# Attention in groups of 64 tokens, two tokens to a row, in units of two batches and half the heads

## The reference

```python
# r, k, v: (4 batches, 8 heads, 768 tokens, 48), w, u: (8, 48)
for t in range(S):                                   # linear attention with a decaying state
    kt, vt, rt = (k[:, :, t], v[:, :, t], r[:, :, t])
    cur = np.einsum('bhd,bhe->bhde', u[None] * kt, vt)
    y[:, :, t] = np.einsum('bhd,bhde->bhe', rt, state + cur)
    state = w[None, :, :, None] * state + np.einsum('bhd,bhe->bhde', kt, vt)
x = y.transpose(0, 2, 1, 3).reshape(B * S, H * D)    # 3072 x 384
# soft mixture of experts: 8 experts, 4 slots each
logits = x @ phi                                     # 3072 x 32
d = softmax over the tokens; slot_input = d.T @ x    # 32 x 384
slot_out[e] = np.maximum(slot_input[e] @ w1[e], 0.0) @ w2[e]
x = softmax over the slots of logits @ slot_out
# feed-forward: elu between two matrices
h = x @ w_in                                         # 3072 x 2048
g = np.where(h > 0.0, h, np.exp(np.minimum(h, 0.0)) - 1.0)
out = g @ w_out                                      # 3072 x 384
```

## Time and profile before

| | |
|---|---|
| median of 3 runs | 399.86 us (398.61 to 400.44) |
| profiled execution | 397.44 us, its span 395.7 us |
| PE busy | 377.8 us, 95% of the span |
| DVE, ACT, POOL busy | 267.8, 220.0, 105.1 us |
| DMA | 87,280 packets, 51.80 MB; 77,776 packets under 512 bytes |
| chain that ended last | PE 77%, SP's queue 12%, DMA 3%, issue 3% |

### The profile page before, as it was taken

One profiled execution on the slowest core, in us unless ns is written; L12 is line 12 of the kernel. 1 busy time (PEld: TensorE's weight loads), 2 busy tenths in 40 slices (PEclk: granted clock), 3 DMA queues, 4 the chain that ended last, 5 costly groups with the idle time before them and its releaser, 6 DMA issues.

```text
span 395.7 us, 11454 instructions
## 1 busy us (share of the span) xinstructions
PE 377.8 (95%) x4379; PEld 335.1 (85%) x4379; DVE 267.8 (68%) x514; ACT 220.0 (56%) x499; POOL 105.1 (27%) x136
## 2 busy tenths in 40 slices
PE   6898999999969999999999999999999999999997
PEld 3787898988855453489999999999999999999996
DVE  3787788777756820499966776677767776677671
ACT  2796778777763140468664446444654465455541
POOL 5897877777640000146400000000000000000000
PEclk9999999999999999999999999999999999999999
DMA  9998899999999999830011002000200020002002
GB/s 173 226 170 187 179 224 230 236 258 253 257 328 432 396 385 404 328 80 2 0 36 47 2 0 80 0 0 0 80 0 0 0 80 0 0 0 81 1 2 80
DMA packets 87280, 51.80 MB, mean 131 GB/s; under 512 B 77776, under 2 KB 83024, under 8 KB 85200
## 3 DMA queue, kind: packets, MB, share of 16 engines
q1 hardware_dynamic: 82912, 50.40, 42.9%
q10 hardware_dynamic: 4336, 0.98, 1.3%
HBM read 45.86 MB, written 4.72 MB: 128 GB/s over the span
## 4 chain that ended last, share of the span: by engine, by line
PE 77%; SPq 12%; DMA 3%; issue 3%; DVE 2%; POOL 2%; ACT 0%; POOLq 0%; DVEq 0%
PE psum L969 17%; PE psum L971 17%; PE psum L970 16%; PE psum L905 6%; SPq L367 5%; SPq L369 3%; PE psum L836 3%; SPq L368 3%; PE psum L817 3%; DMA r_raw<-in_r_dram 3%; PE psum L594 2%; PE psum L634 2%; PE psum L677 2%; PE psum L687 1%; PE psum L658 1%
## 5 line engine op out<-in xcount | busy, mean ns | idle before, releaser
L971 PE MATMUL psum<-w_out_hi,elu_lo 128*128 128x384 f32 x372 | 125.8, 338 | 0.0
L969 PE MATMUL psum<-w_out_hi,elu_hi 128*128 128x384 f32 x372 | 125.7, 338 | 0.0
L970 PE MATMUL psum<-w_out_lo,elu_hi 128*128 128x384 f32 x372 | 125.3, 337 | 0.0
L1398 ACT ACTIVATE exp_h<-psum 128x512 f32<-128x512 f32 x96 | 57.7, 601 | 100.5 <-PE psum L905 100.4
L1245 DVE SCALAR_TENSOR_TENSOR elu<-psum,neg_part 128x512 f32<-128x512 f32 x96 | 66.2, 690 | 57.1 <-ACT neg_part L1385 57.1
L970 PEld LDWEIGHTS psum<-w_out_lo,elu_hi 128*128 128x128 f32 x372 | 69.8, 188 | 3.8
L969 PEld LDWEIGHTS psum<-w_out_hi,elu_hi 128*128 128x128 f32 x372 | 70.4, 189 | 0.0
L971 PEld LDWEIGHTS psum<-w_out_hi,elu_lo 128*128 128x128 f32 x372 | 69.9, 188 | 0.0
L1237 DVE TENSOR_TENSOR elu_lo<-elu,elu_hi 128x512 fp32r<-128x512 f32 x96 | 67.0, 698 | 0.6
L1279 ACT ACTIVATE scores<-ident_wide,bonus 128x128 f32<-128x128 f32 x192 | 58.8, 389 | 6.1 <-DVE bonus L1021 5.9
L1385 ACT ACTIVATE neg_part<-exp_h 128x512 f32<-128x512 f32 x96 | 59.9, 626 | 1.7 <-DVE elu L1245 1.3
(11 more groups left out here) (158 smaller groups left out, 410.7 us busy)
## 6 DMA issues: line engine op xcount, KB each, us to landing
w<-in_moe_w_dram SPq DMA_DIRECT2D x8, 1536.0 KB, 10.5
w_sb<-in_moe_w_dram SPq DMA_DIRECT2D x8, 1024.0 KB, 6.0
out_dram<-out_sb SPq DMA_DIRECT2D x24, 192.0 KB, 1.9
w_sb<-in_moe_w_dram SPq DMA_DIRECT2D x8, 512.0 KB, 6.4
w_out_raw<-in_moe_w_out_dram SPq DMA_DIRECT2D x4, 768.0 KB, 12.4
r_raw<-in_r_dram SPq DMA_DIRECT2D x12, 192.0 KB, 3.2
r_raw<-in_r_dram SPq DMA_DIRECT2D x24, 96.0 KB, 3.7
w_in_sb<-in_moe_w_in_dram SPq DMA_DIRECT2D x1, 2304.0 KB, 17.2
```

The source lines that it names most:

```text
L969: pe.matmul(acc, hi, w_out_hi[:, f, :], start=(f == 0), stop=False)
L970: pe.matmul(acc, hi, w_out_lo[:, f, :], start=False, stop=False)
L971: m = pe.matmul(acc, lo, w_out_hi[:, f, :], start=False, stop=(f == KF2 - 1))
L1398: act.activation(exp_h[:, f % 2, :], banks[4 + f % RING][:, :], ACT.Exp).then_inc(exp_done, 1)
```

## The change

Chunks stay at 128 tokens, units at 24. What a unit is changes: two batches of one chunk and four of the eight heads (`pr` is the pair of batches, `half` the half of the heads). A partition row holds two neighbouring tokens of one batch, 64 rows for each of the two batches, so a row of a transfer is 2 x 48 numbers, 384 bytes, and `load` issues two DMAs instead of three. Inside a chunk each batch is cut into two groups of 64 tokens, 32 rows each; with two batches there are four groups in a unit, one for each quarter of the partitions (`GROUPS`, `GROUP` = 32). Scores are 64 x 64 tokens per group and head, half as many elements as before. The second group of a batch must then see a state that has the first group in it: `state_mid`, made by DVE from the old state and the first group's key values (`state_middle`), and `state_sum` for the chunk's end (`state_end`).

Since tokens 2i and 2i+1 lie in one row, sums over tokens are two matmuls, one for each (`q`), and since a group has 32 rows its matmuls use tiles of 32 rows or 32 columns. `key_values`, `attend` and `values` are 32 matmuls a unit each, `state_in` comes in two parts of 8. r is turned by 16 matmuls with the identity on tiles of 64 rows (`turn_raw`) instead of 4 transposes, and waits for its part of PSUM; k is turned by 4 transposes as before. PSUM is laid out anew: banks 0 to 3 hold y and the key values, one bank for each group, 4 and 5 hold the turned r and the scores, 6 k, 7 x.

The diagonal moves from ACT to DVE (`diagonals`, one product of 512 columns), the copy of x from DVE to ACT, the decay from POOL to ACT (`decayed`). The copy of y on ACT is two instructions. The rows of the output lie two tokens apart, and each block of 128 is stored with two DMAs. The experts and the feed-forward stage have the same instructions on other banks.

```diff
+        GROUP = HP // 2
+        Q = 2
+        HALF_H = H // 2
...
-        v_sb = place("v_sb", [P, 2, B, H // 2, HP], F32)
-        scores = place("scores", [P, 2, H, P], F32)
+        v_sb = place("v_sb", [P, 2, H, Q * D], F32)
+        scores = place("scores", [P, 2, 2, 2, Q, HP], F32)
...
-        LOADED = 3 * 16
+        LOADED = 2 * 16
...
-        def load(eng, out, x, c, g, loaded):
-            bs, t0 = slice(2 * g, 2 * g + 2), c * P
-            even, odd = (x[rev, bs].rearrange("b t i d -> t b i d") for rev in range(2))
-            eng.dma_start(out[:, 0, bs, :, 0:D], even[t0:t0 + P]).then_inc(loaded[g], 16)
-            eng.dma_start(out[0:HP, 1, bs, :, 0:D], odd[t0 + HP:t0 + P]).then_inc(loaded[g], 16)
-            eng.dma_start(out[HP:P, 1, bs, :, 0:D], odd[t0:t0 + HP]).then_inc(loaded[g], 16)
+        def load(eng, out, x, c, pr, loaded):
+            for b in range(2):
+                eng.dma_start(out[b * HP:b * HP + HP, pr], x[2 * pr + b, c]).then_inc(loaded[pr], 16)
...
+            def turn_raw(out, raw, pr, half):
+                for a in range(2):
+                    for q in range(Q):
+                        for b in range(2):
+                            for two in range(2):
+                                rows = slice(b * HP, b * HP + HP)
+                                m = pe.matmul(out[rows_of(two), b, Q * a + q, :],
+                                              raw[rows, pr, head(half, two, a), q * D:(q + 1) * D],
+                                              ident[rows, rows], start=True, stop=True, skip_group_check=True)
+                return m
...
+                for a in range(2):
+                    for q in range(Q):
+                        for g in range(GROUPS):
+                            for two in range(2):
+                                rows, toks = rows_of(two), slice(g * GROUP, (g + 1) * GROUP)
+                                m = pe.matmul(ps_A[toks, two, a, q * HP:(q + 1) * HP], k_pair[rows, half, a, q, toks],
+                                              r_pair[rows, half, a, :, toks], start=True, stop=True,
+                                              skip_group_check=True)
+                m.then_inc(A_done, 1)
...
+            def key_values(un, pr, half, c, last):
...
+                pe.wait_ge(v_loaded[pr], LOADED * (c + 1))
+                wait_for(pe, yT_ready, un)
+                pe.nop(nofuse=True)
+                for a in range(2):
+                    for q in range(Q):
+                        for g in range(0, GROUPS, 2 if last else 1):
+                            for two in range(2):
...
+            def state_in(un, b, half, first, last, part):
+                if part == 0:
+                    pe.wait_ge(mid_ready, un + 1)
+                    if not first:
+                        pe.wait_ge(state_ready, un - B + 1)
+                    if not last:
+                        pe.wait_ge(state_summed, un + 1)
+                else:
+                    pe.wait_ge(inter_half_done, un + 1)
...
+            def values(un, pr, half, first):
+                pe.wait_ge(scores_ready, un + 1)
+                pe.wait_ge(inter_done, un + 1)
...
-                        key_values(un, b, i, c, 2 if first and b == 0 else un + 1)
-                    if not (first and b == 0) and not (last and b == B - 1):
-                        turn_k(un + 1, 1 - i, un + 2)
-                        turn_r(un + 1, (b + 1) % B, c + (b + 1) // B)
...
+                        turn_k(un + 1, 1 - half)
+                    key_values(un, pr, half, c, last)
...
+                        turn_r(un + 1, (b + 1) % B // 2, 1 - half, c + (b + 1) // B)
+                    state_in(un, b, half, first, last, 0)
+                    if not (first and b == 0):
+                        turn_x(un - 1, (b - 1) % B // 2, 1 - half)
...
+                    state_in(un, b, half, first, last, 1)
+                    values(un, pr, half, first)
+                    if not final:
+                        attend(un + 1, 1 - half)
...
+            def state_end(un):
+                dve.wait_ge(mid_ready, un + 1)
+                wait_for(dve, state_ready, un)
+                dve.tensor_tensor(state_sum[:, :, :, :].rearrange("p b a d -> p b (a d)"),
+                                  state_mid[:, un % 2].rearrange("p b a d -> p b (a d)"), ps_kv[:, 1], ALU.add
+                                  ).then_inc(state_summed, 1)
```

More of the change, by code:

```diff
@@ L498, in _ @@
[L498 to L502 removed]
+            pool.memset(phi_sb[:, :, :], 0.0).then_inc(cleared, 1)
+            pool.memset(k_nat[:, :, :, :, :, D:HP], 0.0).then_inc(pads_set, 1)
@@ L626, in attend @@
                 pe.nop(nofuse=True)
-                for cols, first in ((slice(0, P), 0), (slice(HP, P), 1)):
-                    for n in range(2):
-                        for two in range(2):
-                            for half, a in ((0, n + 2 * first), (1, n + 2 - 2 * first)):
-                                rows, e0 = slice(two * HP, two * HP + D), half * HP
-                                m = pe.matmul(ps_A[two][e0:e0 + HP, a, cols], k_pair[rows, i, a, e0:e0 + HP],
-                                              r_pair[rows, i, a, cols], start=True, stop=True, skip_group_check=True)
@@ new lines, in state_in @@
+            def state_in(un, b, half, first, last, part):
[5 more added lines that the diff above has]
+                        pe.wait_ge(state_summed, un + 1)
+                else:
+                    pe.wait_ge(inter_half_done, un + 1)
+                pe.nop(nofuse=True)
+                for s in ((1,) if first else (0, 1)):
+                    for a in range(2):
+                        for two in range(2):
+                            batch = two if part == 0 else 1 - two
+                            g = 2 * batch + s
+                            x = state[rows_of(two), b, batch, a, :] if s == 0 else state_mid[rows_of(two), half, batch, a, :]
+                            m = pe.matmul(banks[g][rows_of(a), two * HP:(two + 1) * HP], x,
+                                          r_pair[rows_of(two), half, a, :, g * GROUP:(g + 1) * GROUP],
+                                          start=(part == 0), stop=False, skip_group_check=True)
+                m.then_inc(inter_half_done if part == 0 else inter_done, 1)
@@ L662, in values @@
-            def values(un, b, i, first, part):
-                if part == 0:
-                    pe.wait_ge(scores_ready, 2 * un + 2)
-                else:
-                    pe.wait_ge(y_half_done, un + 1)
-                pe.nop(nofuse=True)
-                for q_is_half, cols in ((True, slice(0, P)), (False, slice(HP, P))):
-                    for half in range(2):
-                        two = half if part == 0 else 1 - half
-                        q = half if q_is_half else 1 - half
-                        for e in range(2):
-                            h, rows = 2 * (2 * q + e) + two, slice(half * HP, half * HP + HP)
-                            m = pe.matmul(ps_y[e * HP:e * HP + HP, two, q * P + cols.start:q * P + P],
-                                          v_sb[rows, q, b, 2 * e + two, :], scores[rows, i, h, cols],
-                                          start=(first and part == 0 and q_is_half),
-                                          stop=(part == 1 and not q_is_half), skip_group_check=True)
-                m.then_inc(y_half_done if part == 0 else y_done, 1)
@@ L683, in turn_x @@
-            def turn_x(un, b):
+                        for a in range(2):
+                            for g in range(GROUPS):
+                                rows = slice(g * GROUP, (g + 1) * GROUP)
+                                m = pe.matmul(banks[g][rows_of(a), two * HP:(two + 1) * HP],
+                                              v_sb[rows, pr, head(half, two, a), q * D:(q + 1) * D],
+                                              scores[rows, half, two, a, q, :],
+                                              start=(first and g % 2 == 0 and q == 0 and two == 0), stop=(q == Q - 1),
+                                              skip_group_check=True)
@@ L769, in attend_chunk @@
[L769 to L778 removed]
+                        if first and b == 0:
+                            pe.wait_ge(pads_set, 1)
```

639 lines of the change are left out of this document (315 added, 324 removed).

## The result

The changed kernel takes 553.62 us (median of 4 runs, 548.07 to 554.81) against 400.15 us for the kernel before beside it (4 runs, 398.61 to 403.45): 1.379 times as long, 95% interval 1.367 to 1.392. 545 was predicted, with a range of 447 to 575. The profiled execution took 553.66 us, its span 551.9.

A forecast was written before the change was run, and what follows sets the result against it. PE's own work bounds attention before; after, fetching PE's code in blocks of about 243 records at 4.9 us does. From 397.4 us, +148 for attention, +0.6 for stores and -1 behind it gave 545 us, range 447 to 575.

The forecast's parts named there:

- The count: PE's matmuls and weight loads up to the end of attention: 12,740 records after the change, against 5,326 before.
- The price of a block: In attention, each fetched block of about 243 PE records takes 4.9 us, with ends of 4.4 and 5.3.
- The loop not kept: PE's attention loop of 2,178 records is fetched anew each round; attention +148 us; chance 0.52, 519 to 567 us.
- the second case: Rival: PE's attention loop stays in place after all, attention ends at 190 us, total 466; chance 0.27.
- The jumps: Three jumps back in PE's attention loop, into the middle of a block, cost 1.5 blocks.
- The matmuls beside the blocks: In attention, PE's own matmuls take 2.1 us in each block of 4.9 us, so the block sets the pace.
- no doubled overlap: Rival, blocks not the pace: small attention tiles without doubled overlap, three times 0.60 us more a unit, total 448; rival's chance 0.12.
- Under half: Sign of being right: PE is busy for under half of attention.
- half the clock: In attention, half the clock makes a block's matmuls 4.2 us instead of 2.1, still under the block, hardly changing it.
- DMA: Loads of r, k and v in attention with 384-byte rows: 0 to -3 us, taken 0, as the blocks cover it.
- The stores: Output stores at the end, eight issues instead of four: 0 to +1.3 us, taken +0.6.
- The stage behind: Experts and feed-forward behind attention lose their own competition for the DMA engines: 0 to -3 us, taken -1.

The follow-up runs named there:

- b_cut408: The kernel before with attention's scores matmuls cut into pieces of 32 columns, values and the state's part into pieces of 64; 484.7 and 494.0 us.
- b_cut568: The kernel before with attention's scores, values and state's part matmuls all cut into pieces of 32 columns; 614.88 us, ratio 1.552.
- a_less: The changed kernel with r turned by 8 wider matmuls and, from chunk 1 on, no second token in scores, key values and values; 443.68 us, ratio 1.112.

## Why the prediction was right, step by step

*The count* held: 12,740 records, and the trace has as many from PE's first matmul to the end of attention.

*The price of a block*, taken as 4.9 us from the two shortest intervals before, is 4.88 where nothing jumps and 4.81 with the loop. It is not a constant, though: 3.98 us a packet in a round of b_cut408, 4.39 without traffic, 5.2 in a round of b_cut568.

*The loop not kept* was the decision, at 0.52 against 0.27, and is shown three times over: ten packets a round in after, none in a_less, and before's own loop falling out when it is cut to 408. Had it been kept, the second case's 466 would have been near, by a_less's rounds of 20.1 us against the 19.6 taken; no run shows the full layout with its loop kept.

The Trainium skill, "Runtime: NRT & Kernel Launch", section "Instruction fetch mechanics", has PE's instruction memory hold 2,048 instructions, in blocks of 256. The forecast leaned on it and came out right, but as a limit for a loop's body the figure doesn't hold: one of 1,757 instructions is fetched anew in each round, and one of 1,373 is not. As the size of the memory it is not refuted: a round of b_cut408 takes nine blocks, and 2,048 instructions are eight. The blocks agree, by the counts of 256. That a branch out of the window must fetch its target agrees too, with stops of 4.23 to 5.17 us at the heads of the rounds; that this window is of two pages doesn't, for bodies of about four and five blocks are kept. That a crossing is "mostly hidden" does not agree, with a stop of 1.83 us in the middle of a group.

*The jumps* were mis-sized: 1.5 blocks, 7 us, were allowed for the three of them, and they cost 15.7 us. Against that the straight code took 50 packets and not 50.7 blocks, and began at 14.6. Together they give 274.8 for the end of attention instead of 270, which is a good half of what the sum was short of.

*The matmuls beside the blocks* were mis-sized too. "2.1 us of matmuls in a block" is given without its working; the prediction's own 4.27 us a unit over 2.17 blocks is 2.0, and it rests on 0.60 us for 64 matmuls on tiles of half the size. The timeline of after at 209.8 to 211.6 us, at a granted clock of 1.00, has 64 of the values from 209.81 to 210.80 and 64 scores in 0.79 us:

```profile
209.81 1.06 PE L704 MATMUL psum<-scores,v_sb 32*48 32x64 f32 x64
210.80 0.86 PE L647 MATMUL psum<-r_pair,k_pair 48*32 48x64 f32 x64
211.59 0.66 PE L633 MATMUL psum<-ident,k_nat 128*128 128x128 f32 x4
```

So 0.99 and 0.79 stand between my 0.60 and the 1.20 of no doubled overlap. The Trainium skill, "TensorEngine Tiling (Array Packing)", sections "Available Configurations" and "Key Properties", lists eight tiles of 32 x 64 and says that tiles work in parallel; the trace agrees with part of that gain and not with all of it. A block then holds 2.36 us of busy PE at full clock and 3.5 to 4.0 at half, and PE is busy for 180 of 260 us. "Under half", the first sign that the prediction named, is wrong. It did not matter here because the block is longer still, but the margin was thin, and b_cut568 shows what happens without it. That half the clock would hardly change the time held as far as whole rounds go, and attention grew when added work brought the clock up; single blocks, as said above, point to some cost.

*DMA*, 0, can't be parted from the rest: that traffic adds 0.4 us a block is measured, what 384-byte rows save in it is not. Nor was the chip asked what the new waits cost with the full layout in place.

*The stores* were mis-sized by more than their range: +0.6 taken, up to 1.3 allowed, 3.0 measured. The reason is in the tile view of the outputs' last issues, before and after (minimum, median, maximum in ns):

```profile
L471 SPq DMA_DIRECT2D out_dram<-out_sb x4: 332/337/343, 391.7 to 393.3; - x4
```

```profile
L494 SPq DMA_DIRECT2D out_dram<-out_sb x8: 482/597/605, 544.9 to 549.3; - x8
```

The 1.91 us for four was the pace of the copies, as the prediction said, with issues of 0.34; four more of these are the 1.3 that it allowed. What it didn't have is that an issue now takes 0.60. Now there are eight of these in a row, and the last one starts 2.85 us after the last copy has ended. *The stage behind*, -1, gave nothing.

In sum: 148 became 153.3, 0.6 became 3.0, -1 became -0.1, and 545 became 553.7.

## What to carry to other kernels

Count an engine's instructions before tiling finer: a matmul in f32 that isn't a transpose is four of them here, and where code must be fetched, here 256 instructions in 4 to 5 us, smaller tiles buy nothing. Look at the packets of the instruction queue in one later round of a loop: none means the loop is kept, and one that isn't is better written out, as far as this one shows. When issues of a queue are priced, take the duration of one from its own rows, and ask whether the change alters it; a merged line of a timeline shows only the pace of what they waited for.

## What the runs showed of the hardware that I had not expected

- PE's loop is kept with 1,314 matmul and load records, 1,373 instructions in all (no packet in a round), and not with 1,698, or 1,757 (nine packets); nothing between was tried. PE's stops lie 256 of its instructions apart, or a multiple of it.
- A jump back to code that is gone costs 5.2 us on average in the changed kernel, more than one block of it, and a round takes one to two packets more than its body has blocks (10 for 8.7 blocks in after, 9 for 6.9 in b_cut408).
- The granted clock of a PE that starts and stops with its code falls to 0.50 (1.2 GHz) and comes back to 1.00 (2.4 GHz) within the same round: 0.54 to 0.68 on average over after's loop rounds, 0.60 with the loop written out, 1.00 in all rounds of before. Wide products between the stops brought it to 0.85 over attention.
- The same output rows, stored in two DMAs with rows two tokens apart, take 0.60 us of SP's queue each instead of 0.34 (medians of the last eight and the last four).
